# A chunked delta rule with a MoE behind it: VectorE's and TensorE's work of a steady turn in another order

## The chip, the cores and the metric

The kernel runs on one core of one Trainium2 chip. The metric is the device time of one execution in microseconds (us), the median of several runs.

## The reference

Three stages follow one another. The first is a delta-rule attention with a 48x48 state for each of 4 batches and 8 heads, over 768 steps; the second is a dense MLP; the third sends each row to one of eight experts.

```python
k_n = k / (np.linalg.norm(k, axis=-1, keepdims=True) + 1e-06)
for t in range(S):
    y[:, :, t] = np.einsum('bhd,bhde->bhe', q[:, :, t], state)
    v_old = np.einsum('bhde,bhd->bhe', state, kt)
    state = state + bt[:, :, :, None] * np.einsum('bhd,bhe->bhde', kt, vt - v_old)
...
h = x @ w_in
g = np.maximum(0.01 * h, h)
return (g @ w_out).astype(np.float32)
...
skip_score = x @ w_skip
logits = xc @ w_gate
out[do_compute] = xc + y
```

## The kernel before

The 768 steps are cut into G = 12 groups of 64 steps. Inside a group the recurrence is solved in closed form: Gram matrices of k with itself (`gram_a`) and with q (`gram_p`), the inverse of a triangular matrix (`inverse`, 33 dependent VectorE links a group, each waiting for the one before), and a short scan (`scan_z`, `scan_u`, `scan_z2`, `scan_u2`, `scan_y`, `scan_s`), done in two halves r = 0 and 1. Every number that a matmul reads is split into a high and a low float16 part, by ScalarE (high) and by VectorE or GpSimd (low), and each product takes three matmuls. The 256 finished rows of a group go through the MLP, which has 16 blocks of the hidden width: `up` (9 matmuls into `b_h`, L646) and `down` (6 into `b_acc`, L659). Between them stand `hidden` (ScalarE, L916), `leaky` (VectorE, L1267), `hidden_high` (ScalarE, L803 on stage) and `hidden_low` (GpSimd, L1574).

All engines run the same loop of turns, `turn(g)` for g from 0 to 12, and each turn has 16 parts, f = 0 to 15. The order inside a part is written out by hand on each engine, and semaphores tie the engines. Turns 1 to 8 hold the same work; in the last ones some of it is missing, since there is no later group to prepare. A part holds one `up` and one `down`. In turn g, part f from 10 on, `up` works on group g and `down` lags two parts behind it. `up` of a part needs the `leaky` of two parts before (semaphore `g_ready`). Beside that a turn does:

- the scan of group g in parts 0 to 6. `scan_z(r)` is followed by VectorE's sum (L1218), ScalarE's high part, VectorE's low part `scan_z_low` (L1223), and then by `scan_u(r)` on TensorE in part 1, which needs that low part and the inverse in `tT` too (`t_loaded`);
- the gate of group g - 1, whose result `x2` the `rows_out` of part 11 writes: three transposes for each half w (`gate_x`, L671), a high and a low part of them in one buffer `x2T` (ScalarE L803, VectorE `gate_x_low`, L1129), and 9 small matmuls (`gate_s`, L684);
- for group g + 1: `gram_p` in parts 10 to 13, with VectorE's mask one part later (L1159, tile pm), the ScalarE copy `p_high` and GpSimd's `p_low`; `inverse_low` in part 12 (L1210), after which SyncE's queue stores the inverse to DRAM (`inverse_out`, L424) and loads it back in another layout (`inverse_back`, L434, eight transfers);
- for group g + 2: `kn_high` and `kn_low` in parts 0 to 2 (L1557 on GpSimd), `gram_a` in 6 to 9, and `q_high` on ScalarE and `q_low` on VectorE (L1129, tile nq);
- for group g + 3: `squares` of k (ScalarE, L813), `norm_sum` (VectorE, L1136), `root` (ScalarE, L817) and `norm` (VectorE, L1140 to L1148, all on 16 columns), and then `nat_k` on GpSimd (L1549), which scales k.

The 33 links of the inverse are dealt over the parts by a table, `SHARE`; half of a part's links (rounded up) stand ahead of `leaky`, the rest behind. Link 0 is L1183, link 1 is L1186, link 2 is L1189; the others alternate between L1197 and L1203. `SECOND` is the table for turn 0.

Of the kernel before, what the change touches and what calls it, by code (L numbers as in the profile page):

```python
# [19 lines left out]
def build(nc, q, k, v, beta, w_in, w_out, w_skip, w_gate, w1, w2, out):  # L20
# [38 lines left out]
    with ctx:  # L59
# [283 lines left out]

        SHARE = (2, 0, 1, 1, 3, 4, 4, 4, 4, 4, 3, 1, 0, 0, 0, 2)

# [199 lines left out]
        def _(pe):  # L545
# [157 lines left out]
            def turn(g):  # L703
                scan, nxt, ahead, gate = is_group(g), is_group(g + 1), is_group(g + 2), is_group(g - 1)
                scans = (scan_z, scan_u, scan_z2, scan_u2, scan_y, scan_s)
                for f in range(FT):
# [16 lines left out]
                    if (g, f) in ((G - 1, 10), (G, 5)):  # L723
                        ranks(g - G + 1)
                    if gate and f == 13:
                        gate_x(g - 1, 0)
                    if gate and f == 14:
                        gate_s(g - 1, 0)
                        gate_x(g - 1, 1)
                    if gate and f == 15:  # L730
                        gate_s(g - 1, 1)

# [68 lines left out]
        def _(act):  # L801
# [165 lines left out]
            def turn(g):  # L967
                scan, nxt, ahead = is_group(g), is_group(g + 1), is_group(g + 2)
                gate, third = is_group(g - 1), is_group(g + 3)
                for f in range(FT):  # L970
                    if scan and f in (1, 3, 4, 6):
                        {1: scan_z, 3: scan_z2, 4: scan_u2, 6: scan_s}[f](g, 1)
                    if scan and f == 5:
                        scan_y(g, 1)
                    if gate and f in (14, 15):
                        gate_x(g - 1, f - 14)
                    if scan and f in (8, 9):
# [24 lines left out]
                    if ahead and f in (0, 1):  # L1002
                        kn_high(g + 2, f)
                    if ahead and f in (13, 14):
                        q_high(g + 2, f - 13)
                    if nxt and f == (11 if g else 12):
                        inverse_high(g + 1)
                    if third and f == 10:
                        squares(g + 3)
                    if third and f == 12:  # L1010
                        root(g + 3)
# [108 lines left out]
        def _(dve):  # L1120
            links = [0]

            def link(i):
                links[0] += 1
                i.then_inc(small, 1)
                dve.wait_ge(small, links[0])
# [11 lines left out]
            def norm(g):  # L1138
                dve.wait_ge(root_ready, g + 1)
                link(dve.tensor_scalar(sm[:, 2, :], sm[:, 1, :], 1e-30, None, ALU.max))  # L1140
                link(dve.reciprocal(sm[:, 3, :], sm[:, 2, :]))
                link(dve.tensor_tensor(sm[:, 4, :], sm[:, 0, :], sm[:, 3, :], ALU.mult))
                link(dve.tensor_tensor(sm[:, 2, :], sm[:, 4, :], sm[:, 1, :], ALU.add))
                link(dve.tensor_scalar(sm[:, 3, :], sm[:, 2, :], 0.5, 1e-6, ALU.mult, ALU.add))
                link(dve.reciprocal(sm[:, 4, :], sm[:, 3, :]))
                if g:
                    dve.wait_ge(nat_ready, g)
                dve.tensor_scalar(sm[:, 5, :], sm[:, 4, :], -K_S, None, ALU.mult).then_inc(norm_ready, 1)  # L1148

# [146 lines left out]
            def turn(g):  # L1296
# [4 lines left out]
                for f in range(FT):  # L1301
# [12 lines left out]
                    if inv and mid > at:  # L1314
                        inverse(n, at, mid)
                    if gate and f in (14, 15):
                        gate_x_low(g - 1, f - 14)
                    if scan and f - 1 in lows:
# [9 lines left out]
                    if scan and f in lows:  # L1328
                        lows[f](g, 0)
                    if ahead and f in (14, 15):  # L1330
                        q_low(g + 2, f - 14)
                    if nxt and f == 4:
                        a21_low(g + 1)
                    if nxt and f == (12 if g else 13):
                        inverse_low(g + 1)
                    if third and f == 11:
                        norm_sum(g + 3)
                    if third and f == 13:
                        norm(g + 3)
# [193 lines left out]
        def _(pool):  # L1533
# [43 lines left out]
            def turn(g):  # L1577
                scan, nxt, ahead = is_group(g), is_group(g + 1), is_group(g + 2)
                for f in range(FT):
                    if g and ahead and f == 0:  # L1580
                        nat_k(g + 2)
                    if ahead and f in (1, 2):
# [5 lines left out]
                    if up_at(g, f):  # L1588
                        hidden_low(*up_at(g, f))
                    if g == G - 2 and 7 <= f < 11:  # L1590
                        constants(f - 7)
# [126 lines left out]
```

## Time and profile before

| | |
|---|---|
| median of 3 runs | 983.75 us (982.42 to 985.75) |
| the profiled execution | 983.13 us, span 981.4 us |
| PE (TensorE matmul) busy | 815.8 us, 83% |
| DVE (VectorE) busy | 680.5 us, 69% |
| ACT (ScalarE) busy | 505.0 us, 51% |
| POOL (GpSimd) busy | 424.8 us, 43% |
| mean granted TensorE clock | 0.932 of 2.4 GHz |

The span is the time from the first to the last instruction of one profiled execution; its own time lies 1.7 us above the span and 0.6 us below the median. A busy share is a mean over stages with different limits: what counts is which engine another one waits for, and where. A granted clock of 1.00 is 2.4 GHz, of 0.50 is 1.2 GHz.

### The profile page before, as it was taken

Reading aid. Unit: us, or ns where it says so; the run is one execution under the profiler, and the core shown is the slowest. Engines: PE = TensorE matmul, PEld = TensorE weight load, DVE = VectorE, ACT = ScalarE, POOL = GpSimd, SP = SyncE. Lnnn points to the kernel's source line nnn. Section 1 sums busy time; section 2 is a strip of 40 time slices with the busy share of each in tenths; the row PEclk is TensorE's granted clock in tenths of the full one; section 3 lists DMA queues with packets and bytes.
Section 4 is the critical chain, followed back from the end, with each engine's and each line's share of the span. In section 5 each row is a group of like instructions: output and inputs, shape, how many; then the busy total and the mean of one; then the engine's idle time right before and its main releaser. Section 6 shows DMA issues by size and latency. Waiting matters only on the chain.

```text
span 981.4 us, 27909 instructions
## 1 busy us (share of the span) xinstructions
PE 815.8 (83%) x10858; PEld 652.6 (67%) x10859; DVE 680.5 (69%) x1318; ACT 505.0 (51%) x1096; POOL 424.8 (43%) x501
## 2 busy tenths in 40 slices
PE   0325879898989989898988889999991989999996
PEld 0224658686767768686767768778771767788865
DVE  5478778787878788787878788785557754633372
ACT  5435556565665756565665656645542724421161
POOL 4403343535444443525344454343332565644463
PEclk9755889999999999999999999999996999999999
DMA  9675536484546656374654555332271861631100
GB/s 240 129 199 86 107 71 116 92 135 88 113 92 119 111 105 124 71 139 84 123 108 100 109 100 109 72 60 55 50 258 43 333 229 38 228 118 48 40 20 18
DMA packets 309830, 109.97 MB, mean 112 GB/s; under 512 B 284930, under 2 KB 301364, under 8 KB 309344
## 3 DMA queue, kind: packets, MB, share of 16 engines
q1 hardware_dynamic: 304000, 94.63, 45.0%
q0 software_dynamic: 3232, 7.64, 2.2%
q10 hardware_dynamic: 2496, 6.29, 1.8%
q8 instruction: 69, 1.13, 0.5%
q14 instruction: 33, 0.27, 0.1%
HBM read 60.39 MB, written 20.46 MB: 82 GB/s over the span
## 4 chain that ended last, share of the span: by engine, by line
PE 48%; DVE 23%; ACT 9%; issue 8%; DMA 5%; SPq 3%; POOL 2%; DVEq 0%; POOLq 0%; ACTq 0%
PE b_h L646 11%; PE b_acc L659 10%; PE b_acc L785 8%; PE b_h L769 7%; PE b_ch L584 6%; DMA natq<-x_dram,id_in 3%; DVE stage L1267 3%; ACT z L803 2%; PE b_gr L550 2%; DVE inv L1210 2%; DVE a_sys L1189 2%; DVE z L1223 2%; ACT inv L803 2%; DVE pm L1159 2%; ACT stage L916 2%
## 5 line engine op out<-in xcount | busy, mean ns | idle before, releaser
L1574 POOL TENSOR_TENSOR stage<-stage 128x256 f16<-128x256 f32 x192 | 143.6, 748 | 285.0 <-ACT stage L803 283.4
L646 PE MATMUL b_h<-stage,wt 128*128 128x256 f16 x1728 | 230.3, 280 | 7.1 <-DVE stage L1267 4.8
L659 PE MATMUL b_acc<-wt,stage 128*128 128x384 f16 x1152 | 222.4, 330 | 0.7 <-POOL stage L1574 0.3
L646 PEld LDWEIGHTS b_h<-stage,wt 128*128 128x128 f16 x1728 | 164.9, 100 | 32.1 <-DVE stage L1267 6.0
L803 ACT ACTIVATE stage<-stage 128x256 f16<-128x256 f32 x192 | 80.0, 417 | 132.5 <-DVE stage L1267 132.5
L659 PEld LDWEIGHTS b_acc<-wt,stage 128*128 128x128 f16 x1152 | 108.6, 99 | 58.0 <-issue 3.5
L1267 DVE SCALAR_TENSOR_TENSOR stage<-b_h,stage 128x256 f32<-128x256 f32 x192 | 80.9, 421 | 82.2 <-ACT stage L916 79.4
L785 PE MATMUL b_acc<-wt,operands 128*128 128x384 f16 x576 | 101.6, 326 | 5.9 <-DVE operands L1494 5.9
L769 PEld LDWEIGHTS b_h<-y,wt 128*128 128x128 f16 x1728 | 99.9, 99 | 8.3 <-issue 6.2
L769 PE MATMUL b_h<-y,wt 128*128 128x128 f16 x1728 | 102.5, 221 | 3.2 <-DVE y L1129 2.8
L1564 POOL TENSOR_TENSOR operands<-pm,operands 128x512 f16<-128x512 f32 x48 | 57.3, 1194 | 89.6 <-ACT operands L803 89.6
L916 ACT ACTIVATE stage<-b_h 128x256 f32<-128x256 f32 x192 | 72.6, 378 | 33.7 <-PE b_h L646 33.4
L1203 DVE TENSOR_REDUCE inv<-inv 128x30 f32<-128x90 f32 (+4 forms) x180 | 84.4, 469 | 4.6
L550 PE MATMUL b_gr<-operands 128*128 128x128 f16 x576 | 44.3, 232 | 50.3 <-DMA operands<-operands 21.1
L785 PEld LDWEIGHTS b_acc<-wt,operands 128*128 128x128 f16 x576 | 54.6, 98 | 39.3 <-DVE operands L1494 8.0
L550 PEld LDWEIGHTS b_gr<-operands 128*128 128x128 f16 x576 | 39.3, 104 | 54.6 <-issue 45.3
L1085 ACT ACTIVATE operands<-b_h 128x512 f16<-128x512 f32 x48 | 28.5, 593 | 84.2 <-PE b_h L769 84.1
L1197 DVE TENSOR_TENSOR inv<-a_sys,inv 128x60 f32<-128x60 f32 (+4 forms) x180 | 69.8, 388 | 2.8
L1494 DVE SCALAR_TENSOR_TENSOR operands<-b_h,operands 128x512 f16<-128x512 f32 x48 | 33.0, 688 | 46.0 <-ACT operands L1085 46.0
L584 PE MATMUL b_ch<-z,operands 128*128 128x48 f16 x1152 | 38.4, 186 | 29.7 <-DVE z L1223 26.1
L1129 DVE SCALAR_TENSOR_TENSOR wt<-operands,wt 128x1536 f16<-128x1536 f32 x32 | 56.6, 1777 | 8.1 <-ACT wt L803 7.9
L584 PEld LDWEIGHTS b_ch<-z,operands 128*128 128x128 f16 x1152 | 34.2, 97 | 41.6 <-issue 32.2
(172 smaller groups left out, 1350.7 us busy)
## 6 DMA issues: line engine op xcount, KB each, us to landing
operands<-in_moe_w_dram SPq DMA_DIRECT2D x16, 1536.0 KB, 7.9
a_sys<-a_dram SPq DMA_DIRECT2D x24, 256.0 KB, 3.8
natq<-in_q_dram SPq DMA_DIRECT2D x24, 192.0 KB, 4.0
raw_v<-in_v_dram SPq DMA_DIRECT2D x24, 192.0 KB, 3.6
stage<-y SPq DMA_DIRECT2D x96, 48.0 KB, 2.2
x_dram<-stage SPq DMA_DIRECT2D x24, 192.0 KB, 2.8
out_dram<-stage SPq DMA_DIRECT2D x24, 192.0 KB, 3.0
natk<-in_k_dram SPq DMA_DIRECT2D x22, 192.0 KB, 4.0
```

The source lines that it names most:

```text
L550: mm = pe.matmul(b_gram[st % 2][:, p * P:(p + 1) * P], kT[g % 2][:, a, u, :], rhs[:, b, u, :], start=(p == 0 and (a, b) == PARTS[0]), stop ...
L584: mm = pe.matmul(b_ch[r][:, i * D:(i + 1) * D], lhs[:, a, u, :], rhs[:, b, u * D:(u + 1) * D], start=(first and i == 0 and (a, b) == PARTS ...
L646: mm = pe.matmul(b_h[f % 2][:, 0:GT], wt[0][:, a, d * FF + f * P:d * FF + (f + 1) * P], xT[:, g % 2, b, d, :], start=(i == 0), stop=(i == ...
L659: mm = pe.matmul(b_acc[w][:, 0:DM], g16[:, f % 4, a, w * P:(w + 1) * P], wt[1][:, b, f * DM:(f + 1) * DM], start=(f == 0 and (a, b) == PAR ...
L769: mm = pe.matmul(b_h[half][:, f * P:(f + 1) * P], wt[i][:, a, d * F1 + fc:d * F1 + fc + P], xgT[:, b, d * P:(d + 1) * P], start=(f == 0 an ...
L785: mm = pe.matmul(b_acc[0][:, 0:DM], e16[:, half, a, f * P:(f + 1) * P], wt[i][:, b, w0:w0 + DM], start=(half == 0 and f == 0 and (a, b) == ...
L803: return act.activation(o, i, ACT.Copy, scale=scale)
L916: act.activation(r32[:, f % 2, :], b_h[f % 2][:, 0:GT], ACT.Relu, scale=0.99).then_inc(h_relu, 1)
L1197: dve.tensor_tensor(inv[:, 1:3].rearrange("p k (r i) -> p k r i", i=BLK)[:, :, 0:rows, c:BLK], a[:, c - 2:c, c:BLK].unsqueeze(2).to_broadc ...
L1203: dve.tensor_reduce(t_next[:, 0:rows, c:BLK], planes.rearrange("p k (r i) -> p r i k", i=BLK)[:, 0:rows, c:BLK], AX.X, ALU.add).then_inc(t ...
L1267: dve.scalar_tensor_tensor(g32[:, f % 4, :], b_h[f % 2][:, 0:GT], 0.01, r32[:, f % 2, :], ALU.mult, ALU.add).then_inc(g_ready, 1)
L1574: pool.tensor_tensor(g16[:, f % 4, LO, :], g32[:, f % 4, :], g16[:, f % 4, HI, :], ALU.subtract).then_inc(g_lo, 1)
```

## The change

What is computed stays the same. The change has six parts:

- TensorE transposes x2 in parts 12 and 13 (before: 13 and 14), and the two `gate_s` stay in 14 and 15. ScalarE and VectorE split the transposes in 13 and 14 (before: 14 and 15).
- q's split moves on ScalarE from parts 13 and 14 to 10 and 11, on VectorE from 14 and 15 to 12 and 13.
- `squares` moves from part 10 to 8, `root` from 12 to 10, `norm_sum` from 11 to 9 and `norm` from 13 to 11.
- `norm` has six operations in place of seven: the factor goes into the last but one.
- GpSimd scales k at the end of part 15 of the turn before, in place of part 0.
- `SHARE` deals the 33 links anew. From part 15 on it gave 2, 2, 0, 1, 1, 3, 4, 4, 4, 4, 4, 3, 1 (parts 15, 0 to 11), and now gives 1, 1, 1, 4, 0, 4, 4, 3, 4, 5, 2, 4, 0.

```diff
-        SHARE = (2, 0, 1, 1, 3, 4, 4, 4, 4, 4, 3, 1, 0, 0, 0, 2)
+        SHARE = (1, 1, 4, 0, 4, 4, 3, 4, 5, 2, 4, 0, 0, 0, 0, 1)
...
-                    if gate and f == 13:
-                        gate_x(g - 1, 0)
-                    if gate and f == 14:
-                        gate_s(g - 1, 0)
-                        gate_x(g - 1, 1)
-                    if gate and f == 15:
-                        gate_s(g - 1, 1)
+                    if gate and f in (12, 13):
+                        gate_x(g - 1, f - 12)
+                    if gate and f in (14, 15):
+                        gate_s(g - 1, f - 14)
...
-                    if gate and f in (14, 15):
-                        gate_x(g - 1, f - 14)
+                    if gate and f in (13, 14):
+                        gate_x(g - 1, f - 13)
...
-                    if ahead and f in (13, 14):
-                        q_high(g + 2, f - 13)
+                    if ahead and f in (10, 11):
+                        q_high(g + 2, f - 10)
...
+                    if third and f == 8:
+                        squares(g + 3)
                     if third and f == 10:
-                        squares(g + 3)
-                    if third and f == 12:
                         root(g + 3)
...
-                link(dve.tensor_scalar(sm[:, 3, :], sm[:, 2, :], 0.5, 1e-6, ALU.mult, ALU.add))
-                link(dve.reciprocal(sm[:, 4, :], sm[:, 3, :]))
+                link(dve.tensor_scalar(sm[:, 3, :], sm[:, 2, :], -0.5 / K_S, -1e-6 / K_S, ALU.mult, ALU.add))
                 if g:
                     dve.wait_ge(nat_ready, g)
-                dve.tensor_scalar(sm[:, 5, :], sm[:, 4, :], -K_S, None, ALU.mult).then_inc(norm_ready, 1)
+                dve.reciprocal(sm[:, 5, :], sm[:, 3, :]).then_inc(norm_ready, 1)
...
-                    if gate and f in (14, 15):
-                        gate_x_low(g - 1, f - 14)
+                    if gate and f in (13, 14):
+                        gate_x_low(g - 1, f - 13)
...
-                    if ahead and f in (14, 15):
-                        q_low(g + 2, f - 14)
+                    if ahead and f in (12, 13):
+                        q_low(g + 2, f - 12)
...
+                    if third and f == 9:
+                        norm_sum(g + 3)
                     if third and f == 11:
-                        norm_sum(g + 3)
-                    if third and f == 13:
                         norm(g + 3)
...
-                    if g and ahead and f == 0:
-                        nat_k(g + 2)
...
+                    if is_group(g + 3) and f == 15:
+                        nat_k(g + 3)
```

TensorE, parts 13 to 15 of a steady turn before. The first row is the last `gram_p`; L671 are the transposes of x2 and L684 is `gate_s`.

```order
L550 MATMUL b_ch<-operands 128x128 x12
L671 MATMUL b_tr<-ident,stage 128x128 x3
L646 MATMUL b_h<-stage,wt 128x256 x9
L659 MATMUL b_acc<-wt,stage 128x384 x6
L684 MATMUL b_gr<-wg,stage 128x9 x9
L671 MATMUL b_ch<-ident,stage 128x128 x3
L646 MATMUL b_h<-stage,wt 128x256 x9
L659 MATMUL b_acc<-wt,stage 128x384 x6
L684 MATMUL b_gr<-wg,stage 128x9 x9
```

TensorE at the same place now, from the first transposes in part 12 on:

```order
L671 MATMUL b_tr<-ident,stage 128x128 x3
L646 MATMUL b_h<-stage,wt 128x256 x9
L659 MATMUL b_acc<-wt,stage 128x384 x6
L550 MATMUL b_ch<-operands 128x128 x12
L671 MATMUL b_ch<-ident,stage 128x128 x3
L646 MATMUL b_h<-stage,wt 128x256 x9
L659 MATMUL b_acc<-wt,stage 128x384 x6
L684 MATMUL b_gr<-wg,stage 128x9 x9
L646 MATMUL b_h<-stage,wt 128x256 x9
L659 MATMUL b_acc<-wt,stage 128x384 x6
L684 MATMUL b_gr<-wg,stage 128x9 x9
```

The second half's transposes no longer stand between the two `gate_s`, and between a half's transposes and its `gate_s` lie two parts in place of one.

VectorE, from `leaky` of part 11 to `leaky` of part 13 before (L1267 is `leaky`, L1136 `norm_sum`, L1159 the mask of `gram_p`, L1210 `inverse_low`):

```order
L1267 SCALAR_TENSOR_TENSOR stage<-b_h,stage 128x256
L1136 TENSOR_REDUCE sm<-y 128x16
L1159 TENSOR_TENSOR pm<-b_ch,mask_p 128x512
L1267 SCALAR_TENSOR_TENSOR stage<-b_h,stage 128x256
L1210 TENSOR_TENSOR inv<-inv 128x128x2 x2
L1159 TENSOR_TENSOR pm<-b_gr,mask_p 128x512
L1267 SCALAR_TENSOR_TENSOR stage<-b_h,stage 128x256
```

VectorE now, from `leaky` of part 11 to the mask of part 13 (`leaky` is L1263 here, the mask L1155, `norm` L1137 to L1144, `q_low` L1126, `inverse_low` L1206):

```order
L1263 SCALAR_TENSOR_TENSOR stage<-b_h,stage 128x256
L1137 TENSOR_SCALAR sm<-sm 128x16
L1138 RECIPROCAL sm<-sm 128x16
L1139 TENSOR_TENSOR sm<-sm 128x16
L1140 TENSOR_TENSOR sm<-sm 128x16
L1141 TENSOR_SCALAR sm<-sm 128x16
L1144 RECIPROCAL sm<-sm 128x16
L1155 TENSOR_TENSOR pm<-b_ch,mask_p 128x512
L1263 SCALAR_TENSOR_TENSOR stage<-b_h,stage 128x256
L1126 SCALAR_TENSOR_TENSOR nq<-natq,nq 64x16x48
L1206 TENSOR_TENSOR inv<-inv 128x128x2 x2
L1155 TENSOR_TENSOR pm<-b_gr,mask_p 128x512
```

`norm` now stands ahead of part 12's mask, and `q_low` ahead of `inverse_low` and of part 13's mask.

VectorE, from `leaky` of part 15 to `leaky` of part 1 before (L1186 and L1189 are links 1 and 2, L1129 is `q_low`, L1276 the gate's second result, L1218 and L1223 the scan's sum and low part for the two halves):

```order
L1267 SCALAR_TENSOR_TENSOR stage<-b_h,stage 128x256
L1186 TENSOR_TENSOR inv<-a_sys 128x512
L1129 SCALAR_TENSOR_TENSOR nq<-natq,nq 64x16x48
L1276 TENSOR_SCALAR logit<-b_gr 128x9
L1189 TENSOR_TENSOR a_sys<-a_sys,inv 128x512
L1267 SCALAR_TENSOR_TENSOR stage<-b_h,stage 128x256
L1218 SCALAR_TENSOR_TENSOR scan<-raw_v,b_ch 128x384
L1197 TENSOR_TENSOR inv<-a_sys,inv 128x2x30
L1223 TENSOR_TENSOR z<-scan,z 128x384
L1218 SCALAR_TENSOR_TENSOR scan<-raw_v,b_ch 128x384
L1223 TENSOR_TENSOR z<-scan,z 128x384
L1267 SCALAR_TENSOR_TENSOR stage<-b_h,stage 128x256
```

VectorE at the same place now (links 1 and 2 are L1182 and L1185, the scan's L1214 and L1219):

```order
L1263 SCALAR_TENSOR_TENSOR stage<-b_h,stage 128x256
L1272 TENSOR_SCALAR logit<-b_gr 128x9
L1182 TENSOR_TENSOR inv<-a_sys 128x512
L1263 SCALAR_TENSOR_TENSOR stage<-b_h,stage 128x256
L1214 SCALAR_TENSOR_TENSOR scan<-raw_v,b_ch 128x384
L1219 TENSOR_TENSOR z<-scan,z 128x384
L1214 SCALAR_TENSOR_TENSOR scan<-raw_v,b_ch 128x384
L1185 TENSOR_TENSOR a_sys<-a_sys,inv 128x512
L1219 TENSOR_TENSOR z<-scan,z 128x384
L1263 SCALAR_TENSOR_TENSOR stage<-b_h,stage 128x256
```

`q_low` is gone from part 15, link 1 has moved behind the gate's result into part 0, and link 2 from ahead of part 0's `leaky` to between the two halves of the scan's first step.

## Rows read from the trace of the kernel before

**Rows 1.** Waits of TensorE, 170 to 750 us: us in total, times, longest.

```profile
PE b_gr L684 <- DVE stage L1129: 26.4, 12, 3.1
PE b_ch L584 <- DVE z L1223: 17.6, 17, 1.8
```

**Rows 2.** Windows: us, busy time of each engine, granted clock (PEclk), DMA share.

```profile
346.15:348.07 1.92, 1.92 (x10) 1.36 (x9) 1.92 (x4) 1.74 (x3) 1.78 (x2) 0.50 0.50 47
349.66:404.28 54.62, 49.45 (x708) 39.54 (x705) 43.67 (x90) 33.54 (x81) 24.21 (x25) 0.97 0.55 108
```

**Rows 3.** Timeline, TensorE: start us, us, instructions, idle before.

```profile
340.41 1.15 PE L646 MATMUL b_h<-stage,wt 128*128 128x256 f16 x9
341.40 1.14 PE L659 MATMUL b_acc<-wt,stage 128*128 128x384 f16 x6
345.24 0.38 PE L684 MATMUL b_gr<-wg,stage 128*128 128x9 f16 x9 [2.70 <-DVE stage L1129]
...
346.15 2.13 PE L646 MATMUL b_h<-stage,wt 128*128 128x256 f16 x9
...
349.66 1.14 PE L646 MATMUL b_h<-stage,wt 128*128 128x256 f16 x9
...
355.53 0.76 PE L584 MATMUL b_ch<-z,operands 128*128 128x48 f16 x24 [1.56 <-DVE z L1223]
...
357.80 0.76 PE L584 MATMUL b_ch<-z,operands 128*128 128x48 f16 x24 [0.53 <-DVE z L1223]
...
617.99 0.38 PE L684 MATMUL b_gr<-wg,stage 128*128 128x9 f16 x9 [1.86 <-DVE stage L1129]
...
673.64 0.78 PE L584 MATMUL b_ch<-z,operands 128*128 128x48 f16 x24 [0.24 <-DMA operands<-t_dram]
```

**Rows 4.** Timeline, VectorE, of the turn of Rows 3.

```profile
334.13 0.43 DVE L1267 SCALAR_TENSOR_TENSOR stage<-b_h,stage 128x256 f32<-128x256 f32 x1 [0.78 <-ACT stage L916]
...
337.57 1.68 DVE L1210 TENSOR_TENSOR inv<-inv 128x256 f16<-128x256 f32 x2
339.17 0.68 DVE L1159 TENSOR_TENSOR pm<-b_gr,mask_p 128x512 f32<-128x512 f32 x1
341.76 0.42 DVE L1267 SCALAR_TENSOR_TENSOR stage<-b_h,stage 128x256 f32<-128x256 f32 x1 [1.91 <-ACT stage L916]
...
344.03 0.69 DVE L1159 TENSOR_TENSOR pm<-b_ch,mask_p 128x512 f32<-128x512 f32 x1
...
345.68 0.42 DVE L1267 SCALAR_TENSOR_TENSOR stage<-b_h,stage 128x256 f32<-128x256 f32 x1 [0.50 <-ACT stage L916]
346.02 1.40 DVE L1129 SCALAR_TENSOR_TENSOR nq<-natq,nq 64x768 f16<-64x768 f32 x1
...
351.78 1.65 DVE L1189 TENSOR_TENSOR a_sys<-a_sys,inv 128x512 f32<-128x512 f32 x1
...
354.82 0.56 DVE L1223 TENSOR_TENSOR z<-scan,z 128x384 f16<-128x384 f32 x1 [0.46 <-ACT z L803]
...
356.43 1.22 DVE L1223 TENSOR_TENSOR z<-scan,z 128x384 f16<-128x384 f32 x1 [0.59 <-ACT z L803]
```

**Rows 5.** Timeline, ScalarE: `squares` in part 10.

```profile
332.00 0.83 ACT L813 ACTIVATE y<-natk 128x768 f32<-128x768 f32 x1
```

**Rows 6.** Timeline, GpSimd: `nat_k` and the first `kn_low`.

```profile
350.70 2.19 POOL L1549 TENSOR_TENSOR natk<-natk,sm 128x768 f32<-128x768 f32 x1
...
355.60 1.64 POOL L1557 TENSOR_TENSOR operands<-natk,operands 64x768 f16<-64x768 f32 x1 [0.63 <-ACT operands L803]
```

**Rows 7.** Timeline, all engines, turn 10: `inverse_low` and its load back.

```profile
661.15 1.68 DVE L1210 TENSOR_TENSOR inv<-inv 128x256 f16<-128x256 f32 x2
...
665.79 6.10 SPq L434 DMA_DIRECT2D operands<-t_dram  x8
```

**Rows 8.** Timeline, SyncE's queue, the turn of Rows 3.

```profile
326.67 1.34 SPq L382 DMA_DIRECT2D natq<-in_q_dram  x2
...
342.19 5.34 SPq L434 DMA_DIRECT2D operands<-t_dram  x8
```

## The prediction

> **What bounds the kernel now.** I read the waits of TensorE first. It is the busiest engine, and over the stretch of the turns its idle time goes mostly to two places: 26.4 us before `gate_s`, for VectorE's `gate_x_low`, and 17.6 us before `scan_u`, for `scan_z_low` [rows 1]. Then I read one turn in the timelines. A steady turn lasts 54.62 us, at a mean granted clock of 0.97 [rows 2].
>
> The first wait: `down` of part 14 starts at 341.40, takes 0.98 like the `up` before it (340.41 to 341.40), and `gate_s` starts at 345.24 [rows 3]. Behind that idle time the clock is at 0.50, 1.2 GHz [rows 2], and an `up` shows 2.13 in place of 1.15. The `up` of part 0 starts at 349.66 [rows 3]. At full clock and with no wait, part 14's `up` at 340.41 would be followed by four blocks of 0.98, two `gate_s` of 0.24 and 0.33 of transposes: 345.1. So wait and low clock cost 4.5 us a turn. The second wait: `scan_u` starts at 355.53 and 357.80, after 1.56 and 0.53 of idle time [rows 3].
>
> What is late is VectorE and ScalarE in turns. `inverse_low` (337.57) holds back the mask of part 13 (339.17); behind that come ScalarE's `p_high`, the seed of the next inverse and `hidden`, so that `leaky` of part 13 starts at 341.76, 2.59 behind the mask. Then come `norm` and part 14's mask (344.03), and `gate_x_low` behind it releases TensorE at 345.24 [rows 3, 4].
>
> **The change, part by part.** I take the same turn, in the clock of its rows, and let TensorE run unhindered up to part 12.
>
> *Parts 8 to 11.* VectorE gets one link more ahead of part 8's `leaky` (some 0.5), ScalarE gets the 0.83 of `squares` [rows 5] there, and q's split in 10. Part of it is made good, since `norm_sum` is gone from part 11. For `leaky` of part 11 (334.13) I take 334.75, bounds 334.13 and 335.6 (both additions in full). TensorE feels nothing: `up` needs `leaky` only two parts, some 5 us, later.
>
> *Parts 11 to 13.* `norm` follows. From `leaky` at 341.76 to the mask at 344.03 are 2.27, of which `leaky` holds 0.34 (345.68 to 346.02) [rows 4], so the seven operations take 1.93; with one small one fewer I take 1.73. The mask of part 12 then starts at 334.75 + 0.34 + 1.73 = 336.8. From a mask to the next `leaky` without a seed are 1.65 (344.03 to 345.68), here some 0.15 more because ScalarE also has `rows_out`, q's second half and `inverse_high` before it: `leaky` of part 12 at 338.6. Now `q_low` (1.33 of its 1.40 before the next can start) and `inverse_low` (1.60, 337.57 to 339.17): the mask of part 13 at 338.6 + 0.34 + 1.33 + 1.60 = 341.9. That is 2.7 later than before. From there, as before, 2.59 to `leaky` of part 13: 344.5.
>
> *What TensorE meets.* It comes to part 14's `gate_s` at 342.7, since both transposes now stand ahead. `gate_x_low` follows its mask and ends 1.2 behind that mask's start (as 344.03 to 345.24): 343.1, a wait of 0.4 in place of 2.7. But `up` of part 15 needs `leaky` of part 13: it could start at 343.35 and starts at 344.9, a **new wait of 1.55**. Behind `leaky` stand `q_low`'s second half (1.33) and the mask of part 14 (344.5 + 0.34 + 1.33 = 346.2), then 1.65 to `leaky` of part 14 at 347.85; on it waits `up` of part 0, at **348.25 in place of 349.66**. So of the 4.5 us only 1.4 come back here: the q split and `norm` have moved ahead of `inverse_low`, and what waited in one piece now waits in four. If the clock falls all the same, as it did behind 1.86 of idle time at 617.99 [rows 3], the slow `up` and `down` lie mostly inside waits that are there anyway, and I estimate 0.3.
>
> *Parts 0 and 1.* Before, `q_low` and link 2 (1.65) kept VectorE from the scan's sum. Now only link 0, link 1 and two `leaky` stand there. `leaky` of part 0 starts at 350.7, sum, high part and low part follow (together 1.9), and `scan_u` starts at 352.7: 4.4 behind `up` of part 0, where it was 5.9. Then link 2 comes between the halves. It takes 1.65 beside `nat_k` (350.70 for 2.19, rows 4 and 6). The second low part took 1.22 beside `kn_low`, the first 0.56 with GpSimd idle [rows 4, 6]. So the second `scan_u` comes between 354.9 (both fast) and 356.5 (both slow); I take 355.6, against 357.80. Some 0.15 is lost again behind the four links of part 2, which lie between scan steps.
>
> The sharing of SBUF by the two engines works against this step in one more place. `nat_k` no longer ends before the first low part, but overlaps it. The Trainium skill, GPSIMD Engine Reference, section Specifications, says that GpSimd contends with VectorE instructions that have two SBUF inputs, and `scan_z_low` is one. The 1.22 against 0.56 above agrees. By the rule the first low part would take up to 0.66 longer, which would make a turn's gain 1.4 where the sum has 2.05.
>
> *The inverse's way through DRAM.* `inverse_low` starts at 340.3 in place of 337.57, while `scan_u` starts 2.8 sooner. In turn 10 `inverse_low` started at 661.15 and `scan_u` waited for the load until 673.64 [rows 3, 7]: 12.5 us, or 11.7 with the 5.34 that the queue takes for the eight loads in a steady turn [rows 8] in place of 6.10. That gives 352.0 to 352.8 against 352.7: just hidden. In turn 0, where VectorE has the second table's links in parts 10 to 12 too, `norm` and both q halves push `inverse_low` back by about 4 us, and the first scan of turn 1 waits for the load; I put 1.0 of loss.
>
> *GpSimd* does `nat_k` at practically the same moment as before, behind the last `hidden_low`; the cover is that `kn_high` comes only behind the scan's high part. Loads of q and k: q's data are needed 9 us sooner. In the turn shown the queue issues that load from 326.67 to 328.0 [rows 8]. The last small load of the inverse was issued until 671.9 and used at 673.64, 1.7 later [rows 3, 7]; q's load is bigger, and I allow 4, so 332.0. ScalarE comes to the split about 0.8 after the place where `squares` stood (332.00, rows 5): 332.8, just behind it.
>
> **The sum.** Turns 1 to 8: 357.80 - 355.6 - 0.15 = 2.05, less some for the clock: 2.0 each, 16.0. Turn 9 has q and no `norm`: its wait is 1.86 [rows 3], and I take 1.9. Turn 10 loses 0.35 to the added link ahead of part 9's x split, where `up` waits for it. With turn 0: 16.0 + 1.9 - 0.35 - 1.0 = 16.5. The profiled execution took 983.13, so 966.6; the median of the runs is 0.6 above it: **967**, taken as 966.5. The per-turn bounds are 1.2 (part 11 late by 0.8 more, the second low part slow) and 2.9 (no lateness in part 11, all fast): 974 to 958.
>
> **The rivals.**
> *The whole wait goes.* If `leaky` of part 13 came in time, only the load of the inverse would bound: `inverse_low` at about 338.9 gives `scan_u` at 350.6 to 351.4, 4.1 to 4.9 a turn, some 36 us: 947. For it speaks that the transposes are split a part sooner; against it, that the 1.55 comes out of durations with hardly a gap between them. 9%.
> *The wait only moves.* If ScalarE's queue in parts 8 to 11 adds another 1.4 us, or q's data land that late, `up` of part 0 starts at 349.66 again, with the clock low; what is left is part of the scan's gain: 0.5 a turn or less, 979 to 983. For it speaks that ScalarE gets `squares` and q's split where it has four Gram copies; against it, that it is busy only 33.5 of 54.6 us [rows 2]. 10%.
> *Slower: the load of the inverse becomes the chain.* It decides once `inverse_low` starts so late that 12.5 us later lies behind 355.53, so after 343.0, 2.7 later than I forecast. Each us beyond costs one in all eight turns: at 345.5, 20 us more, 1003. For it: everything that moved stands ahead of `inverse_low`, and turn 10 shows the wait. Against it: it needs twice the slip I find. 6%.
>
> **How the numbers follow.** My forecast, 958 to 974, has 73%, the rivals 9, 10 and 6; 2 are for what I don't see. About 0.3%, 3 us, is what a measurement tells from no change. Faster: 73 + 9 and half of the second rival, 0.87; within 0.3%: 0.06; slower: 0.07. The range that leaves out 2 in 10 reaches from 954, part of the way to the first rival, to 977.
>
> **What would show it.** `gate_s` waits 0 to 0.8 us a turn in place of 2.7; `up` of part 15 shows a wait of 1 to 2 us for L1263, that of part 0 another of about 0.6; the first `scan_u` waits under 0.6, the second 0.5 to 1.5; a steady turn lasts 52.6 us. In the rows of VectorE the mask of part 13 starts some 7.1 us behind `leaky` of part 11, in place of 5.0 [rows 4]. I am wrong if the wait for `leaky` is missing (then the first rival), if `scan_u` waits for t_dram in every turn (the third), or if ScalarE reaches `hidden` of part 11 more than 1.5 us later than before in its turn (the second).

## The result and the profile after

The changed kernel takes 966.57 us (median of 4 runs, 965.62 to 969.27), the kernel before, measured beside it, 984.0 us (982.42 to 985.75). The ratio is 0.983, 95% interval 0.982 to 0.985. Measured again later beside other kernels (e12), the same kernel gave 970.56 us and 0.986 (0.9835 to 0.988); where two of its profiles differ is told with that run. The profiled execution took 966.15 us, its span is 964.4.

TensorE's waits from 170 to 750 us, the view of [rows 1] (us in total, times, longest):

```profile
PE b_h L646 <- DVE stage L1263: 12.9, 9, 1.5
PE b_ch L584 <- DVE z L1219: 7.4, 8, 1.3
...
PE b_gr L684 <- DVE logit L1272: 5.6, 8, 1.4
PE b_acc L659 <- POOL stage L1570: 3.4, 10, 0.4
PE b_ch L584 <- DMA operands<-t_dram: 2.6, 4, 0.8
...
PE b_gr L684 <- DVE stage L1126: 0.8, 1, 0.8
```

The 26.4 us before `gate_s` for the split are 0.8, the 17.6 us of the scan are 7.4, and in their place stand four that were not there or came to 0.2 us: `up` for `leaky`, the second `gate_s` for VectorE's reading of the first (logit), `down` for `hidden_low`, and the scan for the inverse's load.

A turn in the windows, the view of [rows 2], and the stretch behind TensorE's wait in it:

```profile
296.97:349.58 52.61, 49.57 (x702) 39.20 (x703) 42.79 (x89) 33.04 (x81) 23.50 (x25) 0.97 0.62 111
340.04:341.93 1.89, 1.89 (x6) 0.82 (x7) 1.38 (x5) 1.24 (x4) 1.02 (x1) 0.50 0.47 44
```

From the second `scan_u` of turn 1 to that of turn 9 go (559.41 - 139.54) / 8 = 52.48 us a turn, before (576.76 - 139.26) / 8 = 54.69. The clock fell to 1.2 GHz behind the wait in two of the eight turns, in place of all eight; the turn shown is one of the two. In the six others TensorE's timeline reads like this one, of the turn before:

```profile
286.11 1.16 PE L646 MATMUL b_h<-stage,wt 128*128 128x256 f16 x9 [1.49 <-DVE stage L1263]
287.62 1.15 PE L659 MATMUL b_acc<-wt,stage 128*128 128x384 f16 x6 [0.36 <-POOL stage L1570]
289.37 0.37 PE L684 MATMUL b_gr<-wg,stage 128*128 128x9 f16 x9 [0.60 <-DVE logit L1272]
289.60 1.14 PE L646 MATMUL b_h<-stage,wt 128*128 128x256 f16 x9
...
296.97 0.77 PE L584 MATMUL b_ch<-z,operands 128*128 128x48 f16 x24 [1.25 <-DVE z L1219]
```

The timeline of TensorE in the turn of the windows, as [rows 3]:

```profile
336.64 0.38 PE L684 MATMUL b_gr<-wg,stage 128*128 128x9 f16 x9
338.52 1.16 PE L646 MATMUL b_h<-stage,wt 128*128 128x256 f16 x9 [1.49 <-DVE stage L1263]
340.04 2.10 PE L659 MATMUL b_acc<-wt,stage 128*128 128x384 f16 x6 [0.36 <-POOL stage L1570]
341.93 0.42 PE L684 MATMUL b_gr<-wg,stage 128*128 128x9 f16 x9
342.21 1.70 PE L646 MATMUL b_h<-stage,wt 128*128 128x256 f16 x9
...
347.02 0.76 PE L584 MATMUL b_ch<-z,operands 128*128 128x48 f16 x24
...
349.58 0.76 PE L584 MATMUL b_ch<-z,operands 128*128 128x48 f16 x24 [0.82 <-DVE z L1219]
```

and of VectorE, as [rows 4]:

```profile
328.51 0.42 DVE L1263 SCALAR_TENSOR_TENSOR stage<-b_h,stage 128x256 f32<-128x256 f32 x1 [1.06 <-ACT stage L913]
...
332.63 0.42 DVE L1263 SCALAR_TENSOR_TENSOR stage<-b_h,stage 128x256 f32<-128x256 f32 x1 [1.22 <-ACT stage L913]
...
334.30 1.22 DVE L1206 TENSOR_TENSOR inv<-inv 128x256 f16<-128x256 f32 x2
335.45 0.68 DVE L1155 TENSOR_TENSOR pm<-b_gr,mask_p 128x512 f32<-128x512 f32 x1
...
338.04 0.42 DVE L1263 SCALAR_TENSOR_TENSOR stage<-b_h,stage 128x256 f32<-128x256 f32 x1 [1.45 <-ACT stage L913]
...
341.14 0.42 DVE L1263 SCALAR_TENSOR_TENSOR stage<-b_h,stage 128x256 f32<-128x256 f32 x1 [0.51 <-ACT stage L913]
...
345.85 1.03 DVE L1219 TENSOR_TENSOR z<-scan,z 128x384 f16<-128x384 f32 x1 [0.59 <-ACT z L800]
...
347.26 1.71 DVE L1185 TENSOR_TENSOR a_sys<-a_sys,inv 128x512 f32<-128x512 f32 x1
348.89 0.55 DVE L1219 TENSOR_TENSOR z<-scan,z 128x384 f16<-128x384 f32 x1
```

These are the `leaky` of parts 11, 12, 13 and 14, with the mask of part 13 between, and below them the scan's first low part, link 2 and the second low part. Part 10's `up` starts at 323.38 here and started at 329.57 in the turn of the prediction. Counted from it, in us:

| | forecast | measured |
|---|---|---|
| `leaky` of part 11 | 5.2 | 5.13 |
| `leaky` of part 12 | 9.0 | 9.25 |
| mask of part 13 | 12.3 | 12.07 |
| `leaky` of part 13 | 14.9 | 14.66 |
| `up` of part 15 (TensorE) | 15.3 | 15.14 |
| `leaky` of part 14 | 18.3 | 17.76 |
| `up` of part 0 | 18.7 | 18.83, clock low |
| first `scan_u` | 23.1 | 23.64 |
| second `scan_u` | 26.0 | 26.20 |

Where the 17.0 us between the two profiled spans are, by stretches that begin and end with the same instruction (forecast beside it, where there was one):

| stretch | us | forecast |
|---|---|---|
| start to the second `scan_u` of turn 0 | +1.3 | |
| turn 0 | -1.0 | +1.0 |
| turns 1 to 8 | -17.6 | -16.0 |
| turn 9 | -1.8 | -1.9 |
| turn 10 | +0.4 | +0.35 |
| turn 11 to the experts' first transpose | +0.1 | |
| the experts | +1.6 | |

The first and the last are no work of the change. In the first, ScalarE waited 6.26 us in place of 4.30 for the first load of q; the same stretch took 2.6 us longer than before in e1, which changes nothing in it. The last holds the same instructions.

### The profile page after: what moved, and what is told of

Its sections match the earlier page's. It is cut to its first block, busy times and chain, and to the rows that moved or that the text cites. A ratio compares the mean times of both kernels' runs of the same rounds, so it can differ in the third digit from the quotient of the medians.

```text
span 964.4 us, 27897 instructions
## 1 busy us (share of the span) xinstructions
PE 808.6 (84%) x10858; PEld 646.2 (67%) x10859; DVE 674.3 (70%) x1306; ACT 500.7 (52%) x1096; POOL 423.1 (44%) x501
## 4 chain that ended last, share of the span: by engine, by line
PE 52%; DVE 21%; issue 8%; ACT 8%; DMA 5%; SPq 3%; POOL 2%; DVEq 0%; ACTq 0%; POOLq 0%
PE b_acc L659 13%; PE b_h L646 12%; PE b_acc L782 8%; PE b_h L766 7%; PE b_ch L584 5%; PE b_gr L550 3%; PE b_ch L550 2%; DVE z L1219 2%; DVE inv L1199 2%; DVE stage L1263 2%; DVE inv L1193 2%; ACT stage L913 2%; DMA natq<-in_q_dram 1%; ACT inv L800 1%; DVE nq L1126 1%
## 5 line engine op out<-in xcount | busy, mean ns | idle before, releaser
L1570 POOL TENSOR_TENSOR stage<-stage 128x256 f16<-128x256 f32 x192 | 146.4, 763 | 269.4 <-ACT stage L800 267.8
L646 PE MATMUL b_h<-stage,wt 128*128 128x256 f16 x1728 | 222.0, 274 | 20.0 <-DVE stage L1263 17.5
L646 PEld LDWEIGHTS b_h<-stage,wt 128*128 128x128 f16 x1728 | 159.9, 98 | 41.2 <-DVE stage L1263 19.5
L659 PEld LDWEIGHTS b_acc<-wt,stage 128*128 128x128 f16 x1152 | 106.2, 98 | 62.0 <-POOL stage L1570 8.6
L1263 DVE SCALAR_TENSOR_TENSOR stage<-b_h,stage 128x256 f32<-128x256 f32 x192 | 80.6, 420 | 82.6 <-ACT stage L913 82.4
L1193 DVE TENSOR_TENSOR inv<-a_sys,inv 128x60 f32<-128x60 f32 (+4 forms) x180 | 76.6, 425 | 2.5
L1126 DVE SCALAR_TENSOR_TENSOR wt<-operands,wt 128x1536 f16<-128x1536 f32 x32 | 57.3, 1799 | 8.9 <-ACT wt L800 8.6
L584 PE MATMUL b_ch<-u,operands 128*128 128x48 f16 x1728 | 56.7, 185 | 0.3 <-DVE u L1224 0.3
```

The costliest lines, as they stand in the source:

```text
L584: mm = pe.matmul(b_ch[r][:, i * D:(i + 1) * D], lhs[:, a, u, :], rhs[:, b, u * D:(u + 1) * D], start=(first and i == 0 and (a, b) == PARTS ...
L646: mm = pe.matmul(b_h[f % 2][:, 0:GT], wt[0][:, a, d * FF + f * P:d * FF + (f + 1) * P], xT[:, g % 2, b, d, :], start=(i == 0), stop=(i == ...
L659: mm = pe.matmul(b_acc[w][:, 0:DM], g16[:, f % 4, a, w * P:(w + 1) * P], wt[1][:, b, f * DM:(f + 1) * DM], start=(f == 0 and (a, b) == PAR ...
L1193: dve.tensor_tensor(inv[:, 1:3].rearrange("p k (r i) -> p k r i", i=BLK)[:, :, 0:rows, c:BLK], a[:, c - 2:c, c:BLK].unsqueeze(2).to_broadc ...
L1263: dve.scalar_tensor_tensor(g32[:, f % 4, :], b_h[f % 2][:, 0:GT], 0.01, r32[:, f % 2, :], ALU.mult, ALU.add).then_inc(g_ready, 1)
L1570: pool.tensor_tensor(g16[:, f % 4, LO, :], g32[:, f % 4, :], g16[:, f % 4, HI, :], ALU.subtract).then_inc(g_lo, 1)
```

## The experiments

All ratios are against the kernel before, measured beside the run. "The turn" is the mean of turns 1 to 8, from the second `scan_u` of turn 1 to that of turn 9: 54.69 us before, 52.48 in the changed kernel.

### The parts of the change, one alone or one undone

**e1, x2's transposes moved, nothing else.** The three edits on `gate_x` and `gate_x_low` of the diff, in the kernel before.

> The kernel before with only x2's transposes moved (TensorE 12 and 13, the splits 13 and 14). My theory: VectorE and ScalarE form one chain from part 11 to part 1, so the 2.7 us wait before gate_s goes, but TensorE only arrives sooner at scan_u, which q's split and link 2 still hold. From the rows of before, leaky of part 15 comes 0.7 us sooner (one split less ahead of it) and everything behind it too: 0.75 a turn, some 7 us, 977. Rival A, the gate wait and the low clock behind it are the whole cost: 4.4 us a turn go, 945 to 950. Rival B, the gate move is worth nothing alone: 984.

978.92 us, ratio 0.994 (0.992 to 0.996). TensorE's waits, 170 to 560 us:

```profile
PE b_gr L684 <- DVE logit L1273: 18.4, 7, 2.8
PE b_ch L584 <- DVE z L1220: 14.2, 14, 2.6
```

The wait for the split is gone, and 2.6 us stand before the second `gate_s` instead, which needs VectorE to have read the first one's result; that reading has `q_low` in front of it. The scan still waits. So the move that the change is written around is worth 5 us by itself, about a third of the gain; rival A of this run (945 to 950) is out.

**e2, the change without that move.**

> The changed kernel with x2's transposes back in parts 13 and 14 (splits 14 and 15). My theory: q's split and the norm now stand ahead of the split that gate_s waits for; gate_s would wait some 5 us (347.4 against 342.4 in the clock of the turn shown), and the turn is as long as before or longer: 984 to 992. Rival: the shorter scan wait comes from the links and q alone and is kept: 972.

997.1 us, ratio 1.013 (1.010 to 1.017): slower than the kernel before, and by 5 us more than the range I gave. The same view:

```profile
PE b_gr L684 <- DVE stage L1129: 30.3, 7, 4.3
```

With the norm and q's split ahead of it, the split of x2 must be a part sooner, or `gate_s` waits 4.3 us each time.

**e3, the change with the old table of links.**

```diff
-        SHARE = (1, 1, 4, 0, 4, 4, 3, 4, 5, 2, 4, 0, 0, 0, 0, 1)
+        SHARE = (2, 0, 1, 1, 3, 4, 4, 4, 4, 4, 3, 1, 0, 0, 0, 2)
```

> The changed kernel with the old table of links. My theory: link 1 stands ahead of and link 2 right behind the gate's second result, both before leaky of part 0; that leaky comes 1.1 us later, the first scan_u 0.9 later, the second 0.6 later, since nothing lies between the halves: some 5 us, 972. Rival A: the table does nearly all of it, 984. Rival B: it does nothing, 966.6.

964.86 us, ratio 0.980 (0.976 to 0.983). My theory and rival A are both out: the new table gives nothing, and the turn is shorter without it, 51.86 against 52.48. TensorE's timeline of a turn:

```profile
339.34 1.16 PE L646 MATMUL b_h<-stage,wt 128*128 128x256 f16 x9 [1.05 <-DVE stage L1263]
...
348.24 0.76 PE L584 MATMUL b_ch<-z,operands 128*128 128x48 f16 x24 [1.09 <-DVE z L1219]
...
350.21 0.76 PE L584 MATMUL b_ch<-z,operands 128*128 128x48 f16 x24 [0.23 <-DVE z L1219]
```

and three rows of VectorE, link 2 and the scan's two low parts:

```profile
344.65 1.06 DVE L1185 TENSOR_TENSOR a_sys<-a_sys,inv 128x512 f32<-128x512 f32 x1
...
347.10 0.99 DVE L1219 TENSOR_TENSOR z<-scan,z 128x384 f16<-128x384 f32 x1
...
349.14 0.92 DVE L1219 TENSOR_TENSOR z<-scan,z 128x384 f16<-128x384 f32 x1 [0.59 <-ACT z L800]
```

The same two operations in the changed kernel, in a turn at full clock:

```profile
294.22 0.69 DVE L1185 TENSOR_TENSOR a_sys<-a_sys,inv 128x512 f32<-128x512 f32 x1
294.89 1.94 DVE L1219 TENSOR_TENSOR z<-scan,z 128x384 f16<-128x384 f32 x1
```

Two things were mis-sized. Part 15's wait is 1.05 in place of 1.49: with the old table (four links in part 8 in place of five, three in part 10 in place of four) `leaky` of part 11 comes 4.56 us behind `up` of part 10 in place of 5.13. Which entry of the table does it isn't shown. And link 2 costs more between the scan's halves than its place in the table says: there it and the second low part run one behind the other while GpSimd does `kn_low`, and take 2.6 us together (0.69 + 1.94; in the low-clock turn 1.71 + 0.55), where e3 pays 1.06 for the link in part 0 and 0.92 for the low part. The first scan wait is longer in e3, the second shorter, and their sum about the same (1.09 + 0.23 against 1.25). From `up` of part 0 to the first `scan_u` it is 5.40 in place of 4.38, as expected; to the second it is 7.37 in both, where 0.6 more was expected.

**e5, the change without q's move.** Parts 13 and 14, 14 and 15 for `q_high` and `q_low`, as before.

> The changed kernel with q's split back in parts 13 and 14 (ScalarE) and 14 and 15 (VectorE). My theory: the work of VectorE between part 11 and the scan's sum stays the same, and moving q only decides at which of TensorE's waits it shows: the waits for leaky in parts 15 and 0 go, and q's halves (2.7 us) come back ahead of leaky of part 0, so the scan's sum starts where it does now. 966.6, within 3 us. Rival: the earlier q split is what gives the gain, since it leaves the stretch ahead of the scan; then most of the 17 us are lost, 978 or more.

970.64 us, ratio 0.985 (0.983 to 0.987): 1 us outside of what was expected, and not to be told by its time from the change, at 0.983 and 0.986. Its turn is a little longer, 53.05. The 1.5 us at part 15 go down to 0.4 and the wait before the second `gate_s` rises to 1.9. q's place decides where TensorE waits, hardly how long.

**e6, the change without the norm's move.**

> The changed kernel with squares, root, norm_sum and norm back in parts 10, 12, 11 and 13. My theory: the norm (1.7 us) then stands behind leaky of part 13 together with q's second half, and part 14's mask comes 0.6 later than now (346.8 against 346.2 in the clock of the turn shown): up of part 15 no longer waits, that of part 0 waits more, 5 us in all, 971. Rival: moving the norm is worth nothing, because it only trades one wait for another: 966.6.

982.67 us, ratio 0.998 (0.996 to 0.999). Neither fits: against 0.983 and 0.986 the norm's place is worth 12 to 14 us. VectorE's timeline, `leaky` of parts 11 and 12 and the norm's last two operations with part 14's mask:

```profile
337.65 0.42 DVE L1263 SCALAR_TENSOR_TENSOR stage<-b_h,stage 128x256 f32<-128x256 f32 x1 [1.47 <-ACT stage L913]
...
341.76 0.42 DVE L1263 SCALAR_TENSOR_TENSOR stage<-b_h,stage 128x256 f32<-128x256 f32 x1 [2.23 <-ACT stage L913]
...
349.88 0.17 DVE L1141 TENSOR_SCALAR sm<-sm 128x16 f32<-128x16 f32 x1
350.09 0.25 DVE L1144 RECIPROCAL sm<-sm 128x16 f32<-128x16 f32 x1
350.26 0.63 DVE L1155 TENSOR_TENSOR pm<-b_ch,mask_p 128x512 f32<-128x512 f32 x1
```

`up` of part 10 starts at 332.60 here, so `leaky` of part 12 comes 9.16 behind it, with no norm ahead of it: as late as with the norm (9.25). I had put that lateness down to the norm. What holds `leaky` there is `hidden` on ScalarE, which has `rows_out`, q's second half, `inverse_high` and `p_high` before it. So in part 11 the norm lies under a wait that is there anyway, and in part 13 it lies on the chain: part 14's mask comes 17.66 us behind `up` of part 10 (changed kernel: 16.10), and in turns at full clock the wait before the second `gate_s` is 2.18 in place of 0.60.

**e9, the same with ScalarE's second half of q's split a part later.** This tells the two apart.

```diff
-                    if ahead and f in (10, 11):
-                        q_high(g + 2, f - 10)
+                    if ahead and f in (10, 12):
+                        q_high(g + 2, f // 12)
```

> The changed kernel with the norm's four steps back, as before, and with ScalarE's second half of q's split moved on from part 11 to 12. The trace of the version with only the norm back says that leaky of part 12 comes 9.16 us behind up of part 10, as with the new norm (9.25), so it is ScalarE's queue of part 11 (rows_out, q, inverse_high) that holds it, and the norm in part 11 costs nothing because it lies under that queue. Then leaky of part 12 comes about 0.8 sooner here, and the turn with it: 7 to 9 us below the 982.7 of that version, 974. Rival: VectorE sets it, and this does nothing: 982.

973.47 us, ratio 0.990 (0.987 to 0.993), as forecast from ScalarE's queue. `up` of part 10 starts at 328.89, and `leaky` of part 12 comes 8.15 behind it, 1.0 sooner:

```profile
337.04 0.42 DVE L1263 SCALAR_TENSOR_TENSOR stage<-b_h,stage 128x256 f32<-128x256 f32 x1 [1.23 <-ACT stage L913]
```

**e10, the change with `nat_k` back in part 0.**

> The changed kernel with GpSimd's scaling of k back at the start of part 0 of the next turn. On GpSimd only the boundary of the turn lies between the two places, so the order of its work is the same: 966.6, and the same waits.

970.74 us, ratio 0.986 (0.983 to 0.989), with the same waits in the same places and a span of 964.2. This part of the change does nothing.

**e12, the change once more, measured beside e9 to e11.**

> The changed kernel itself, unchanged, for the spread of its time between chips and beside the others of this call: 966.6, ratio 0.983.

970.56 us (968.81 to 975.67, 7 runs), ratio 0.986 (0.9835 to 0.988). Its profiled execution was the slowest of the seven, with a span of 973.9; the turn lasts 52.63, nearly as in the first. One row explains 3.6 of the 9.5 us between the two spans:

```profile
142.58 1.14 PE L584 MATMUL b_ch<-z,operands 128*128 128x48 f16 x24 [5.22 <-DMA operands<-t_dram]
```

The first scan of turn 1 waits 5.22 us for the inverse's load; in the first profile it was 1.52 (137.95), and before the change it did not wait for it at all. Another 2.3 lie before turn 0, and 1.8 in the experts' stage. So the two profiles differ for the most part outside the steady turns. Whether the two medians, 4 us apart, differ for the same reason isn't shown. The parts e5 and e10, at 0.985 and 0.986, are to be compared with both values of the changed kernel, 0.983 and 0.986.

### Further on: what the waits of the changed kernel ask for

**e4, seed later, `inverse_low` sooner.** In the changed kernel ScalarE seeds the next inverse behind `hidden_high` of part 13, and VectorE does `inverse_low` ahead of q's first half.

```diff
-                    if ahead and f == (13 if g else 14):
-                        seed(g + 2)
                     if up_at(g, f):
                         hidden(*up_at(g, f))
...
                         hidden_high(*up_at(g, f))
+                    if ahead and f == (13 if g else 14):
+                        seed(g + 2)
...
-                    if ahead and f in (12, 13):
-                        q_low(g + 2, f - 12)
...
                         inverse_low(g + 1)
+                    if ahead and f in (12, 13):
+                        q_low(g + 2, f - 12)
```

> The changed kernel with two further moves: ScalarE seeds the next inverse behind hidden_high of part 13 in place of ahead of hidden (0.95 us), and VectorE does inverse_low ahead of q's first half in part 12 (the store and load of the inverse start 1.3 us sooner). If the new wait of TensorE at part 15 is what I say, a chain mask, p_high, seed, hidden, leaky, it falls by 0.95 a turn and all behind it comes that much sooner: 8 to 9 us, 958. Rival: the scan of parts 0 and 1 is bound by GpSimd and the links, and takes it back: 965 to 967.

962.97 us, ratio 0.978 (0.975 to 0.981), between the two. The timeline:

```profile
337.58 1.16 PE L646 MATMUL b_h<-stage,wt 128*128 128x256 f16 x9 [0.54 <-DVE stage L1263]
339.43 1.15 PE L659 MATMUL b_acc<-wt,stage 128*128 128x384 f16 x6 [0.69 <-POOL stage L1570]
...
348.80 0.76 PE L584 MATMUL b_ch<-z,operands 128*128 128x48 f16 x24 [1.25 <-DVE z L1219]
```

Part 15's wait fell from 1.49 to 0.54, by the 0.95 of the seed: the chain is shown. 0.33 of it went to `down`'s wait for GpSimd (0.36 in the changed kernel), and the turn is 0.63 shorter, 51.85. The load of the inverse holds the scan in one steady turn, by 0.2.

**e7, that and the old table.**

> The version with the later seed and the earlier inverse_low, with the old table of links. If the old table's 0.6 us a turn and the seed's 0.6 are at different waits (the first at the scan, the second at part 15), they add: 4 to 5 us below the version with the new table in turns 1 to 8, less 1 to 2 lost in turn 0: 959 to 961. If both end at the scan's sum, they don't: 963.

958.09 us, ratio 0.972 (0.970 to 0.974), 1 us better than expected; the turn lasts 51.25. The two add: the old table takes 0.62 from a turn (e3), the seed and `inverse_low` 0.63 (e4), and both together 1.23. This beats both kernels: 27 us below the one before, and below the change by 11 to 13 by the ratios.

**e8, and the first `gate_s` result read a part sooner** (the call of `gate_s(g - 1, 0)` on VectorE moves from the start of part 15 to part 14, ahead of `gate_x_low`).

> The same, and VectorE reads the first gate_s result out of PSUM in part 14, ahead of the second split, in place of behind leaky of part 14; the 0.6 us that TensorE waits there before the second gate_s should go. If nothing else binds, 0.6 a turn or 5 us less than without it, 955; if up of part 0 or the scan's sum then waits for VectorE instead, nothing.

958.39 us, ratio 0.973 (0.971 to 0.974): nothing, by the second branch. The wait for logit is gone, and two others have taken it up:

```profile
340.36 1.16 PE L646 MATMUL b_h<-stage,wt 128*128 128x256 f16 x9 [0.23 <-DVE stage L1263]
346.15 0.77 PE L584 MATMUL b_ch<-z,operands 128*128 128x48 f16 x24 [1.46 <-DVE z L1219]
```

**e11, e7 with the new table for the inverse of turn 0 alone.**

> The version with the old table, the later seed and the earlier inverse_low (958.1), but the inverse that starts in turn 0 is dealt by the new table. Turn 0 to 1 (second scan_u to second scan_u) took 54.8 us there and 53.3 in the changed kernel: if the table makes this difference, 1 to 1.5 us less, 956.8; if not, 958.

958.54 us, ratio 0.974 (0.971 to 0.976). In its profile that stretch took 52.7 against 54.8, but the time is the same as e7's. With a stretch that varies by 3.6 us between two profiles of the changed kernel, the profile of one execution says nothing here; left open.

## Why the prediction was right

*The time and its main term.* 966.6 was forecast for the profiled execution, and it took 966.15. That it is so close is luck: the stretches for which the forecast had a term gave 20.0 us in place of 16.5 (17.6 + 1.8 - 0.4 + 1.0), and 3.0 us that went lost elsewhere, mostly at the start and in the experts, made up for it; measured again, the kernel took 4 us more. The range has a slip too: its terms for the best case (8 times 2.9, and the 0.55 of the other turns) lead to 960, not to 958. The term that carries the forecast, turns 1 to 8 at 2.0 us each, measured 2.2, and the chain behind it holds row by row: the table above differs by at most 0.55 us. In a turn at full clock the way from the second `scan_u` to the next `up` of part 0 is 1.5 us shorter (45.04 for 46.51; 1.4 forecast), and the way from there to the second `scan_u` 0.8 (7.37 for 8.13; 0.65 forecast). `up` of part 15 got the new wait of 1.5, and e4 shows it is the chain mask, `p_high`, seed, `hidden`, `leaky`.

*What part 12's `leaky` waits for* was named wrong: "`norm` follows" and the sum through it gave the right moment (9.0 against 9.25), but e6 has that moment without the norm, and e9 moves it by 1.0 through ScalarE alone. Two chains of nearly one length ended there, and I followed the one that the change touched. The changed kernel's own trace shows which is the longer. VectorE's mask behind the norm, and the last three rows of ScalarE's queue, which has no gap from 328.97 on:

```profile
330.79 0.63 DVE L1155 TENSOR_TENSOR pm<-b_ch,mask_p 128x512 f32<-128x512 f32 x1
```

```profile
331.04 0.77 ACT L800 ACTIVATE inv<-inv 128x256 f16<-128x256 f32 x2
331.71 0.62 ACT L800 ACTIVATE operands<-pm 128x512 f16<-128x512 f32 x1
332.23 0.37 ACT L913 ACTIVATE stage<-b_h 128x256 f32<-128x256 f32 x1
```

The mask is done at 331.42, 0.3 us before ScalarE comes to `p_high`. The price appeared in e6: 971 forecast, 982.67 measured.

*The table of links.* The 0.5 us of the added link in part 8 was in the sum as a cost, and e3 shows one of that size (0.57 at `leaky` of part 11), though not which entry of the table makes it. But I counted the shorter way to the scan as its gain too, and e3 has the same gain without the table. From `up` of part 0 to the second `scan_u` it is 8.13 before, 7.37 in the changed kernel and in e3, and 8.11 in e5, where q is back in parts 14 and 15: that gain is q's. It is partly paid for further up, since e5's turn is only 0.4 to 0.6 us longer. In the sum the table's two effects had not been set against each other.

*The two ends of the scan.* The first `scan_u` came 0.5 later than forecast in the turn of the table, and as forecast in a turn at full clock (4.38 behind `up` of part 0, 293.98 - 289.60). Its low part took 1.03 in the one and 1.01 in the other, in place of 0.56 [rows 4]: in the first with GpSimd's `hidden_low` beside it (345.79 to 346.46, after `nat_k` had ended at 345.83), in the second with `nat_k` until 293.42 and `hidden_low` behind it. The rule on the sharing of SBUF (the Trainium skill, GPSIMD Engine Reference, section Specifications) says that GpSimd contends with VectorE instructions that have two SBUF inputs. The trace agrees, at a place where I had weighed the rule and left it out of the sum. The price is 0.47, below the 0.66 that I had worked out for it (and the 0.56 was not quite alone: `hidden_low` ran beside its first 0.15). At full clock it was made good, since `leaky` of part 0 started 1.76 behind `up` of part 0 (291.36), where I had 2.45.

*The clock.* It stayed at 2.4 GHz in six of eight turns. From `up` of part 15 to `up` of part 0 it is 3.49 us in a turn at full clock (289.60 - 286.11) and 3.69 in the turn shown, where `down` took 2.10 in place of 1.15 but no wait for logit stands behind it. So the low clock costs 0.2 there, and that turn is 0.2 longer than the one before it (52.61 against 52.41); the forecast had 0.3. Before, it cost more. From the first `gate_s` (345.24) to `up` of part 0 (349.66) TensorE took 4.42 without a wait, where the forecast's full-clock figures (two `gate_s`, one half's transposes, `up` and `down`) make 2.77: an estimate of 1.65 us in each of the eight turns. The waits at this place came to 2.70 before and to 2.45 now, so most of what TensorE got back up to part 0 is clock, not waiting.

*Turn 0.* Forecast +1.0, measured -1.0 in one profile and +2.6 in the other. The step (the inverse's load holds the first scan) is right: both profiles show it, at 1.52 and 5.22. Its size hangs on transfers whose time varies.

*The wait that was missing from the forecast* is the second `gate_s` for VectorE's reading of the first, 0.6 a turn. I had a wait of about 0.6 one step later, before `up` of part 0, for `leaky` of part 14; that one is not there. The reading stands right behind this `leaky` on VectorE (341.14 and 341.48), so the forecast had the right chain and the wrong semaphore. e1 shows that the wait can reach 2.6.

*The rivals.* The whole wait did not go, and the inverse's load did not become the chain, though it held the first scan in three turns of 170 to 560 us by 0.6 to 0.8, as the estimate "just hidden" said (in e12 in two of the steady turns, by 0.4 and 1.2); the second `scan_u` came no later for it (7.38 to 7.40 behind `up` of part 0). That the wait only moves came nearest: in a turn at full clock 2.45 us (1.49 + 0.36 + 0.60) stand before `up`, `down` and the second `gate_s` of part 15 for the 2.7 that stood before the first `gate_s`; what went when it moved is most of the low clock behind it.

## What to carry to other kernels

When an operation is moved to a part where its engine waits anyway, it costs nothing, and where that is only shows if one asks for each late event which of the engines' queues is the longer one; two that end within 0.3 us of one another are easily taken for one. A wait of the busiest engine that is taken away alone (e1) comes back at the next semaphore of the same chain; the gain came from moving what stood on the chain off it (e6: 12 to 14 us), and from shortening it at the wait that it then showed (e4: 5 to 8 more by the ratios). Tables that deal filler work should be tested by themselves after each other change: here the old one was better.

## What the runs showed of the hardware

The same VectorE operation changed its duration with what GpSimd did beside it. Link 2 (128x512 float32, two SBUF inputs) took 0.69 us or 1.71 in the same kernel, and the low part behind it (128x384) then 1.94 or 0.55. GpSimd's `kn_low` in the two turns:

```profile
294.50 1.90 POOL L1553 TENSOR_TENSOR operands<-natk,operands 64x768 f16<-64x768 f32 x1
```

```profile
346.78 1.64 POOL L1553 TENSOR_TENSOR operands<-natk,operands 64x768 f16<-64x768 f32 x1 [0.32 <-ACT operands L800]
```

The one that began second paid. Link 2 kept its 0.69 where it began 0.28 before `kn_low`, and `kn_low` took 1.90 in place of 1.64; where it began 0.48 behind `kn_low` (346.78 to 348.42), it ended 0.55 behind it (348.97). The low part that began while `kn_low` ran ended 0.43 behind it (296.83 and 296.40). It reads as if the second waits for the first to end and then does most of its own work; that is a reading of the rows, but the other steady turns of this trace and those of e12 show the same two patterns. In both orders the pair took over 2.2 us. GpSimd's own `nat_k` took 1.48 us in the changed kernel and 2.19 before [rows 6], and `inverse_low` 1.22 and 1.68: a reordering changes the durations from which it was costed.

The clock fell behind idle stretches that look alike. With the wait of 1.49 us at part 15, the `down` that followed took 1.15 in six turns and 1.77 or 2.10 in the other two. The rows don't say what decided.
